# Attention prologue with the fourfold sums taken by TensorE instead of VectorE and GpSimd

## What is computed

```python
def _attn_ref(q, k, v):
    factor = 4
    q_d = q.reshape(B, H, Sd, factor, D).mean(axis=3)
    k_d = k.reshape(B, H, Sd, factor, D).mean(axis=3)
    v_d = v.reshape(B, H, Sd, factor, D).mean(axis=3)
    out_up = np.repeat(sm_attn(q_d, k_d, v_d), factor, axis=2)
    mask = np.abs(pos[:, None] - pos[None, :]) < factor
    out_local = np.matmul(softmax(where(mask, scale * q @ k.T, -1e9)), v)
    return out_up + out_local
# then, with x of 2304 tokens by 512:
#   (silu(x @ w_gate) * (x @ w_val)) @ w_out        512 -> 1536 -> 512
#   h = x @ w_in;  (max(h,0) + alpha*min(h,0)) @ w_out   512 -> 2048 -> 512
```

## Time and profile before

| what | value |
|---|---|
| median of 3 runs | 945.27 us (945.24 to 945.83) |
| the profiled execution's own time | 944.62 us |
| its span in the profile | 942.6 us |
| TensorE busy with matmuls | 925.4 us, 98% |
| TensorE weight loads | 819.2 us, 87% |
| VectorE busy | 503.9 us, 53% |
| ScalarE, GpSimd busy | 275.3 us, 138.9 us |

### The profile page before, as it was taken

One profiled execution on the slowest core, in us unless ns is written; L12 is line 12 of the kernel. 1 busy time (PEld: TensorE's weight loads), 2 busy tenths in 40 slices (PEclk: granted clock), 3 DMA queues, 4 the chain that ended last, 5 costly groups with the idle time before them and its releaser, 6 DMA issues.

```text
span 942.6 us, 18796 instructions
## 1 busy us (share of the span) xinstructions
PE 925.4 (98%) x7752; PEld 819.2 (87%) x7752; DVE 503.9 (53%) x951; ACT 275.3 (29%) x692; POOL 138.9 (15%) x167
## 2 busy tenths in 40 slices
PE   4999999999999999999999999999999999999998
PEld 3899999999999998888899999888888888888886
DVE  8799777545466765453334555444444344444343
ACT  5665444322233433222224432111112111111111
POOL 7876011000011000000016530000000000000000
PEclk9999999999999999999999999999999999999999
DMA  9763323211122222100044430100020020001001
GB/s 271 248 206 98 111 82 103 85 50 41 42 82 97 81 72 86 41 22 14 1 134 134 135 102 1 67 1 0 4 87 1 1 89 2 0 1 45 1 1 45
DMA packets 30691, 63.21 MB, mean 67 GB/s; under 512 B 3344, under 2 KB 10768, under 8 KB 30608
## 3 DMA queue, kind: packets, MB, share of 16 engines
q1 hardware_dynamic: 30608, 62.02, 20.6%
HBM read 52.57 MB, written 9.44 MB: 66 GB/s over the span
## 4 chain that ended last, share of the span: by engine, by line
PE 89%; DVE 1%; issue 0%; ACT 0%; DVEq 0%; ACTq 0%
PE ps L1114 50%; PE ps L1159 21%; PE ps L1142 14%; PE ps L1062 1%; PE ps L998 1%; PE ps L1008 1%; PE ps L1075 1%; PE ps L1046 1%; ACT turned_one L616 0%; DVE v_d_one L784 0%; DVE hidden L946 0%; DVE x_lo L851 0%; DVE y_sb L984 0%; DVE row_max L810 0%; ACT down L598 0%
## 5 line engine op out<-in xcount | busy, mean ns | idle before, releaser
L688 ACT CAST h_hi<-hidden 128x512 fp32r<-128x512 f32 (+4 forms) x152 | 83.2, 548 | 417.9 <-DVE hidden L966 328.1
L1114 PE MATMUL ps<-x_hi,w_hi 128*128 128x416 f32 (+3 forms) x573 | 198.4, 346 | 0.2 <-issue 0.2
L1114 PE MATMUL ps<-x_lo,w_hi 128*128 128x416 f32 (+3 forms) x573 | 192.6, 336 | 0.0
L1114 PE MATMUL ps<-x_hi,w_lo 128*128 128x416 f32 (+3 forms) x573 | 192.5, 336 | 0.0
L930 DVE TENSOR_TENSOR h_lo<-hidden,h_hi 128x512 fp32r<-128x512 f32 (+4 forms) x152 | 109.5, 720 | 67.8 <-ACT h_hi L688 67.8
L963 DVE TENSOR_SCALAR gated<-ps,alpha_sb 128x512 f32<-128x512 f32 (+1 forms) x80 | 55.8, 698 | 162.2 <-PE ps L1114 162.2
L1114 PEld LDWEIGHTS ps<-x_hi,w_hi 128*128 128x128 f32 x573 | 107.6, 188 | 6.6 <-issue 0.5
L1159 PE MATMUL ps<-w_hi,h_hi 128*128 128x512 f32 x288 | 112.2, 390 | 0.0
L1159 PE MATMUL ps<-w_hi,h_lo 128*128 128x512 f32 x288 | 112.2, 390 | 0.0
L1159 PE MATMUL ps<-w_lo,h_hi 128*128 128x512 f32 x288 | 112.0, 389 | 0.0
L1114 PEld LDWEIGHTS ps<-x_hi,w_lo 128*128 128x128 f32 x573 | 107.7, 188 | 4.1
(11 more groups left out here) (141 smaller groups left out, 1341.4 us busy)
## 6 DMA issues: line engine op xcount, KB each, us to landing
w_home<-w SPq DMA_DIRECT2D x68, 256.0 KB, 4.0
qk<-qk SPq DMA_DIRECT2D x30, 436.0 KB, 3.9
vsrc_one<-vsrc SPq DMA_DIRECT2D x58, 144.0 KB
vwin<-vwin SPq DMA_DIRECT2D x30, 192.0 KB, 2.4
x_raw<-y_t SPq DMA_DIRECT2D x4, 1024.0 KB, 6.6
out<-y_sb SPq DMA_DIRECT2D x3, 1024.0 KB, 5.5
y_t<-y_sb SPq DMA_DIRECT2D x2, 832.0 KB, 4.5
y_t<-y_sb SPq DMA_DIRECT2D x2, 576.0 KB, 3.9
```

The source lines that it names most:

```text
L688: nc.scalar.copy(h_hi[r][:, 0:width], hidden[r][:, 0:width]).then_inc(h_hi_ready, 1)
L1114: mm = nc.tensor.matmul(out_ps, w[:, piece, 128 * k:128 * k + 128], x_parts[low][:, k, :], start=(k == 0 and n == 0), stop=(k == KC - 1 an ...
```

## The change

In the prologue alone:

- VectorE averages q only (`average_q`, 288 elements a partition in place of 868). TensorE takes raw k: `first_down_scores` runs over the four neighbours f and accumulates, with keys read at every fourth element. 24 fp32 matmuls in place of six.
- v is not averaged. `pair_outputs` accumulates over the four neighbours with `vsrc` as the weights, read at every fourth element: 32 fp32 matmuls in place of eight. `average_v` of VectorE (pairs 0, 1) and of GpSimd (pairs 2, 3) is gone, and so is the zeroing of three of the four gaps in `vsrc`.
- SyncE loads piece 0 behind v of pair 1, and pieces 1 to 5 behind v of pair 3. The first refill of vsrc now waits for the pair's outputs (`att_ready`) and not for its averages.
- GpSimd normalises all four pairs first and then splits pieces 0 and 1. ScalarE's casts of x and copies are in a slightly different order.

In the first layer's blocks 0 and 1, `average_v` of an overlapped unit stands at place `following + 2`, and ScalarE's cast of a weight piece stands ahead of a unit's step in its place and not behind it.

```diff
-FIRST_LOADS, EARLY_LOADS, LOADS = 3, 16, 7
+FIRST_LOADS, EARLY_LOADS, LOADS = 1, 16, 7
@@ class Unit
+        self.v_averaged = following + 2 if overlapped and following // PLACES < 2 else None
@@ SyncE
             def refill_vsrc(q):
-                sp.wait_ge(v_averaged, q + 1)
                 if q < PAIRS:
+                    sp.wait_ge(att_ready, q + 1)
                     load_vsrc(PAIRS + q, q)
                 elif q + 1 < UNITS:
+                    sp.wait_ge(v_averaged, q + 1)
                     load_vsrc(q + 1, 0)
@@
-            load_pieces(0, FIRST_LOADS)
-            sp.wait_ge(v_gaps_zeroed, POOL_AVERAGES)
+            sp.wait_ge(v_gap_zeroed, 1)
             for k in range(PAIRS):
-                if k == POOL_AVERAGES:
-                    sp.wait_ge(v_gaps_zeroed_pool, PAIRS - POOL_AVERAGES)
                 load_vsrc(k, k)
                 load_vwin(k, k)
+                if k == 1:
+                    load_pieces(0, FIRST_LOADS)
             load_pieces(FIRST_LOADS, EARLY_PIECES)
@@ GpSimd
+            for k in range(PAIRS):
+                normalise(k, k, 0)
             for j in range(POOL_PIECES):
                 split_piece(j)
...
-            normalise(0, 0, 0)
-            normalise(1, 1, 0)
-            average_v(2)
-            normalise(2, 2, 0)
-            normalise(3, 3, 0)
-            average_v(3)
@@ ScalarE, in a place of the first block
                     if has_attention(j):
-                        attention(PLACES * j + p)
                         piece = EARLY_PIECES + p
                         if not j and piece < P1:
                             first_weights_hi(piece)
+                        attention(PLACES * j + p)
@@ VectorE
+            def average_q(k):
+                dve.wait_ge(qk_in[k], 16)
+                nc.vector.tensor_reduce(q_d_early[k][:, :], qk_sb[0][k][:, 0:TB].rearrange("p (s f) -> p s f", f=FACTOR),
+                                        AX_X, ALU.add).then_inc(qk_averaged, 1)
...
-            average_v(0, 0)
             reciprocals(0, 2, 0)
-            average_v(0, 1)
             reciprocals(0, 3, 0)
@@ TensorE
+            def first_down_scores(k):
+                keys = qk_sb[0][k][:, K0:K0 + SEQ].rearrange("p (s f) -> p f s", f=FACTOR)
+                for f in range(FACTOR):
+                    for first in range(0, HQ, GK):
+                        end = min(first + GK, HQ)
+                        for e in range(2):
+                            rows = slice(HEAD * e, HEAD * e + HEAD)
+                            last = nc.tensor.matmul(down_ps(0, k, e)[first:end, :], q_d_early[k][rows, first:end],
+                                                    keys[rows, f, :], start=(f == 0), stop=(f == FACTOR - 1))
+                return last
@@ pair_outputs
-                if mode or k < POOL_AVERAGES:
+                if mode:
                     pe.wait_ge(v_averaged, q + 1)
+                    values = [v_d_one]
                 else:
-                    pe.wait_ge(v_averaged_pool, k - POOL_AVERAGES + 1)
-                for c in range(2):
+                    pe.wait_ge(vsrc_in[k], 16 * TILE_ROWS)
+                    values = [vsrc_sb[0][k][:, :, :, f] for f in range(FACTOR)]
+                steps = [(c, v) for c in range(2) for v in values]
+                for n, (c, v) in enumerate(steps):
```

More of the change, by code:

```diff
@@ L68 @@
 EARLY_HI = 12
-POOL_AVERAGES = 2
+DVE_ZEROES = 2
 BANK = 512
@@ L117, in schedule @@
     for unit, last in zip(units, [None] + units):
-        unit.v_averaged = max(unit.flipped, last.put_out + 1 if last and last.overlapped else 0)
+        if unit.v_averaged is None:
+            unit.v_averaged = max(unit.flipped, last.put_out + 1 if last and last.overlapped else 0)
         unit.outputs_before = PAIRS + sum(u.put_out < unit.scored for u in units)
@@ L189, in build @@
             vsrc_early = [sb(f"vsrc_early{k}", [CHUNK_ROWS, 2, 2 * HEAD, FACTOR], where=early) for k in range(1, PAIRS)]
-            qk_d_early = [sb(f"qk_d_early{k}", [128, AVERAGED], where=early) for k in range(1, PAIRS)]
-            v_d_early = [sb(f"v_d_early{k}", [CHUNK_ROWS, 2, 2 * HEAD], where=early) for k in range(1, PAIRS)]
+            q_d_early = [sb(f"q_d_early{k}", [128, HQ], where=early) for k in range(PAIRS)]
             local_early = [sb(f"local_early{k}", [128, 2 * TILES, GK], where=early) for k in range(1, PAIRS)]
@@ L523, in _ @@
             pool.wait_ge(gaps_zeroed, PAIRS + 1)
-            for k in range(POOL_AVERAGES, PAIRS):
+            for k in range(DVE_ZEROES, PAIRS):
                 nc.gpsimd.memset(turned[0][k][:, :, :, :], 0.0).then_inc(turned_zeroed, 1)
@@ L755, in _ @@
         def _(dve):
[L756 to L758 removed]
+            nc.vector.memset(vsrc_one[CHUNK // GK * GK:TILE_K, :, :, :], 0.0).then_inc(v_gap_zeroed, 1)
+            for k in range(DVE_ZEROES):
                 nc.vector.memset(turned[0][k][:, :, :, :], 0.0).then_inc(turned_zeroed, 1)
@@ L777, in average_v @@
                 q = PAIRS * a + k
-                mode = 1 if a else 0
-                if mode:
-                    dve.wait_ge(vsrc_in[0], 16 * TILE_ROWS * (q - PAIRS + 2))
-                    dve.wait_ge(att_ready, q)
-                else:
-                    dve.wait_ge(vsrc_in[k], 16 * TILE_ROWS)
-                nc.vector.tensor_reduce(v_d[mode][k][:, :, :], vsrc_sb[mode][k][:, :, :, :],
+                dve.wait_ge(vsrc_in[0], 16 * TILE_ROWS * (q - PAIRS + 2))
+                dve.wait_ge(att_ready, q)
+                nc.vector.tensor_reduce(v_d_one[:, :, :], vsrc_sb[1][k][:, :, :, :],
                                         AX_X, ALU.add).then_inc(v_averaged, 1)
@@ L1007, in down_scores @@
                         rows = slice(HEAD * e, HEAD * e + HEAD)
-                        last = nc.tensor.matmul(down_ps(mode, k, e)[first:end, :], qk_d[mode][k][rows, first:end],
-                                                qk_d[mode][k][rows, KD0:AVERAGED], start=True, stop=True)
+                        last = nc.tensor.matmul(down_ps(mode, k, e)[first:end, :], qk_d_one[rows, first:end],
+                                                qk_d_one[rows, KD0:AVERAGED], start=True, stop=True)
+                return last
[8 more added lines that the diff above has]
+                                                    keys[rows, f, :], start=(f == 0), stop=(f == FACTOR - 1))
                 return last
@@ L1032, in pair_scores @@
                     pe.wait_ge(qk_averaged, q + 1)
-                    down_scores(k, mode).then_inc(scores_ready, 1)
+                    first_down_scores(k).then_inc(scores_ready, 1)
             def transpose_down(a, k, mode, overlapped=False, outputs_before=0):
@@ L1074, in pair_outputs @@
                             keys = slice(TILE_K * r, TILE_K * r + CHUNK)
-                            last = nc.tensor.matmul(att_ps(mode, k, r)[rows, DOWN_O:DOWN_O + HQ], v_d[mode][k][keys, c, rows],
-                                                    down_t[mode][k][keys, at:at + HQ], start=(c == 0), stop=(c == 1))
+                            last = nc.tensor.matmul(att_ps(mode, k, r)[rows, DOWN_O:DOWN_O + HQ], v[keys, c, rows],
+                                                    down_t[mode][k][keys, at:at + HQ], start=(n == 0), stop=(n == len(steps) - 1))
                 last.then_inc(att_ready, 1)
```

53 lines of the change are left out of this document (15 added, 38 removed).

## The result

The changed kernel takes **952.11 us**, median of 4 runs (951.17 to 954.93), beside 945.25 us for the kernel before in 4 runs on the same chip (944.32 to 945.83). That is 0.2 us under the 952.3 to 957.4 us of the forecast itself, and inside the whole range only because that takes in rival 1 from 947.5 us on. The steps in between held less well than the total.

The account below looks back on a forecast made before the run. TensorE, busy 98% of the span, bounds the kernel. +9.3 us to the milestone and -0.5 in the first layer gave +8.8 on 944.62, 953.4, plus 0.65 for the median: 954.0 us; forecast 952.3 to 957.4, with rivals 947.5 to 958.5.

Parts of the forecast that it names:

- the forecast itself: Whole kernel: both page waits, with the clock anywhere between its bounds, 952.3 to 957.4 us; chance 0.65.
- rival 1: Scores: second page served as fast as the first, 4.2 us delay, 950.8 us; no page waits, 947.3 us; together chance 0.16.
- the milestone: Prologue's end: first full product group after mode 1's first unit is scored; forecast at 41.1 us against 31.82, +9.3 us.
- I am wrong if the second wait is short: Averaged scores of pair 3: a TensorE "issue" wait of some 7 us was to show; a short one refutes the prediction.
- A pair of scores takes 2.83 us: Scores: eight waves of 0.24 us in place of two add 1.44 us to a pair's 1.39 us.
- The first page stops TensorE in the local scores of pair 2, usable at 13.1: Scores: TensorE reaches instruction 446 at about 10.5 us and waits about 2.6 us for its program page.
- The second page stops it in the averaged scores of pair 3, usable at 23.5, a wait of about 7 us: Scores: the main term; page at instruction 698, asked for at 13.1 us, packet at 20.7, scores end at 25.3.
- Outputs take 11.3 us, with no page in them: After the scores: four outputs of 2.77 us plus transposes of 0.65, 13.7 us at the lower rate, ending at 36.6.
- The clock rises once, at 34.2 us, and halves what is left of the outputs: Outputs: clock rises 10.7 us after dense work begins at 23.5, so the 4.8 us left become 2.4.
- Rival 2: Scores and outputs: reads at every fourth element are slower, up to 0.44 us a wave; 955.4 to 967 us, chance 0.06.
- The tail, 4.5 us: From the end of the outputs to the milestone: 4.5 us, against 5.47 before.
- The first layer, 0.5 us, bounds 0 and 0.9: First layer: moved cast and average touch waits that sum to 0.7 us; credited 0.5 us.

Follow-up runs that it names:

- experiment 1: The change with keys and v read from contiguous slices (wrong elements, same counts and sizes): 952.36 us, ratio 1.0079.
- 2: The change with v averaged again by VectorE and GpSimd, behind GpSimd's four normalisings, and k left on TensorE: 954.28 us, ratio 1.0099.
- experiment 3: The change with q and k averaged by VectorE, only v summed on TensorE: 951.11 us, ratio 1.0061.
- 4: The change with both sums back on VectorE and GpSimd, leaving its loads, order and casts: 944.69 us, ratio 0.9995.
- 5: The kernel before with keys alone summed by TensorE, nothing else changed: 950.78 us, ratio 1.0069.
- 12: The change with sums as before and GpSimd reordered: split piece 0, normalise all pairs, average v, x_lo, piece 1 last: 943.51 us, ratio 0.9977.
- experiments 8 to 11: Kernel before with first-layer edits: both, 942.72 us; cast alone, 942.96; average alone, 944.42; both plus GpSimd normalising pair 2 before averaging its v, 943.40.
- 6: The change with SyncE holding loads from v of pair 2 on until TensorE has scored all four pairs: 949.03 us, ratio 1.0038.
- experiment 7: The change with loads from v of pair 2 on held until all pairs are scored, and contiguous operands: 953.02 us, ratio 1.0068.

## Why the prediction was right, and where not

The sum of the prediction was +9.3 us to the milestone and -0.5 us behind it. It was +8.2 and -1.4. By the sign that the prediction itself named ("I am wrong if the second wait is short") its main term was wrong, and the total came out near because a term of the other sign was missing. Step by step:

- *A pair of scores takes 2.83 us.* Pair 1 takes 2.81 (L1007 at 7.27 and at 10.08), pair 0 2.94. Right, though a wave is 0.28 us and not 0.24, with the other matmuls of pair 1 taking less at the higher level of the clock.
- *The first page stops TensorE in the local scores of pair 2, usable at 13.1.* The place is right; it was usable at 11.72, 1.4 us earlier.
- *The second page stops it in the averaged scores of pair 3, usable at 23.5, a wait of about 7 us.* The place is right. **The size is the term that failed:** 17.91, a wait of 2.5 us. I had carried the delay between entry and packet, 7.9 us, over from the trace of before (20.7 - 13.1 = 7.6 us in the sum), whose packet nobody waited for. In the change it was 3.5 us, less than the 4.2 us of rival 1, which therefore describes the profiled execution better than my forecast. One trace could not tell this delay. For the second page it was 6.2 us in experiment 1, 2.9 in 2, 7.9 in 3, 7.2 in 4, 4.4 in 5 and 6.2 in 12; in experiments 8 to 11, whose TensorE program is that of the kernel before up to there, it was 3.7, 2.5, 8.0 and 7.5 us; and in both kernels with held loads (6 and 7) 1.1 us. With the loads all issued, then, 2.5 to 8.0 us, and the value that I took lies near the top. That this is also why the change's four runs span 3.8 us and those of before 1.5 is likely but not shown.
- *Outputs take 11.3 us, with no page in them.* They took 15.3 us (20.1 to 35.35). This is the second failure, and the more instructive one. I had counted pages up to 698 and stopped; 384 of the 672 new instructions are in the outputs, and edges 1210 and 1465 stopped TensorE there for 1.15 and 1.34 us. A wait of 0.34 us for ScalarE and 1.1 us of the clock's gain that didn't come (next point) make up the rest of the 4.0 us. The failed terms are of opposite sign, -5.2 us in the scores and +4.0 in the outputs. There is a reason for that: where the scores end earlier, the pages of the outputs are waited for, as experiment 3 showed. But the prediction didn't have this reason, so that its total came within 1.9 us was luck as far as the sum goes.
- *The clock rises once, at 34.2 us, and halves what is left of the outputs.* It does not go like that. The granted clock was at its high level already in pair 1, fell in the wait before 17.91, rose again at about 20.2 us, and was low from 30.5 to 40.7 us. TensorE alone, by stretches (length, busy us and matmuls, then the granted clock):

```profile
6.60:16.80 10.20, 7.67 (x271) 1.00 1.05 253
16.90:20.20 3.30, 2.29 (x42) 0.50 1.04 283
20.30:30.40 10.10, 8.48 (x267) 1.00 0.86 294
30.50:40.70 10.20, 8.86 (x181) 0.50 0.47 161
```

  The level of 2.4 GHz from 20.3 to 30.4 us gave the waves with strided v nothing: they stay at 0.13 us there. Only the transposes and the local part ahead of them were faster, 0.9 us (23.74 to 24.63) where at the lower level they take 1.33 (in experiment 3, L1027 at 25.27 to L1059 at 26.60). I had credited 2.4 us; all of TensorE's own work in the outputs came out 1.3 us below the 13.7 us that I gave it at the lower level. The last rise came at 40.8 us, so the nine products of L1109 all ran at 0.24 us apart.
- *Rival 2, strided reads.* At 1.2 GHz they cost 0.02 us a wave, at 2.4 GHz half the speed. The Trainium skill ("SBUF — State Buffer", in the section on the DMA port swizzle) has each access to a new 16-byte line pay a penalty; experiment 1 agrees at the higher clock (0.28 us against 0.15) and hardly shows it at the lower (0.28 against 0.26). It took the outputs' waves most of the clock's gain, which is part of the 1.1 us above. But it doesn't decide the total: experiment 1 was no faster, nor was experiment 7 by its median.
- *The tail, 4.5 us.* It was 4.64.
- *The first layer, 0.5 us, bounds 0 and 0.9.* It was 1.4, outside the bounds. I had taken the waits of the earlier trace rows as all there was to win. From the milestone to the second layer TensorE is idle for 0.2 us where it was 1.2, and its matmuls take 0.4 us less; of what the 0.4 us come is not shown. The cast alone gave 0.24% in 11 runs.

So the direction was right, and so was the kind of mechanism: added matmuls of 9.8 us that don't disappear in the idle time, because TensorE stands for its pages. Its size and its places were not. Two things show the pages at work: in experiment 3 the scores end 7.1 us earlier and the first product starts no earlier, and in experiment 1 shorter waves in the scores are followed by longer page waits and the same total. That ScalarE, VectorE or GpSimd hold TensorE up in the change is excluded by its waits (0.3 us).

Left open: by what the delay of a page is set beyond "much data issued" (for the second page 2.5 to 8.0 us, 1.1 us with held loads; 0.8 us later on, when the queues are quiet), since the rows don't show which queue or ring the packet stands in; and how the 6.9 us would divide if every page came at once, since no kernel here shows the change without its page waits.

## What to carry to other kernels

Count the instructions, not only the columns: at the start of a kernel, while its loads saturate the queues, TensorE got its program at about 250 weight loads and matmuls every 5.4 to 6.2 us wherever it stood for it in the change (6.8 to 10.3 us at times in experiments 1, 3 and 7). Work cut into small tiles ran through a page faster than that, so moving sums onto TensorE there was dear even where TensorE looked idle, and making the tiles faster gained nothing. A delay read from one trace, for a page that nobody waited for, is one draw out of many and no term for a sum. Two halves of such a change are to be tried apart, and small edits elsewhere in it too: here the one worth keeping was the cast that took two lines.

## What the runs showed of the hardware that was not expected

- A stop at a page's edge can recur in steady work: 1.1, 2.5, 1.2 and 1.3 us in the change, up to 6.2 us in experiment 1. The Trainium skill ("Runtime: NRT & Kernel Launch", Instruction fetch mechanics) has an engine execute one page of 256 instructions while the next is fetched, with the crossing mostly hidden. The page size agrees (702 - 446 = 256). Hidden the crossing is behind 40 us in the change, and before that, from instruction 446 on, in one case of five (near 958).
- An fp32 matmul whose moving operand takes every fourth element ran as fast at 2.4 GHz as at 1.2 (0.28 us a wave of 144 columns), where a contiguous one went from 0.26 to 0.15. With every fourth element in the weights, waves of 72 columns took 0.13 us against 0.07, both at 2.4 GHz.
- The granted clock fell twice within 40 us and rose again each time, falling once during a wait of 2.5 us. In experiment 1 it was at 0.50 from 14.2 to 44.8 us, through waits and dense work alike.
